# Routing tokens to experts: one-hot slots shared with ScalarE, row ids by thirds, low halves and put rows moved behind the row ids, and a weight load issued at a step's end

## What is computed

```
logits = (x2 / |x2|) @ (emb / |emb|).T / tau          # 3072 x 8
expert_idx = argmax(logits, axis=1)
gate_w = softmax(logits)[n, expert_idx[n]]
for e in range(8):
    mask = expert_idx == e
    h = maximum(x2[mask] @ w1[e], 0)                  # 384 -> 1024
    out[mask] = gate_w[mask, None] * (h @ w2[e])      # 1024 -> 384
```

## Time and profile before

| | us |
|---|---|
| median of 3 runs | 843.85 |
| lowest and highest run | 841.52, 848.44 |
| the profiled execution's own time | 842.68 |
| span of its profile | 840.9 |

### The profile page before, as it was taken

One profiled execution on the slowest core, in us unless ns is written; L12 is line 12 of the kernel. 1 busy time (PEld: TensorE's weight loads), 2 busy tenths in 40 slices (PEclk: granted clock), 3 DMA queues, 4 the chain that ended last, 5 costly groups with the idle time before them and its releaser, 6 DMA issues. The chain is left out here.

```text
span 840.9 us, 18148 instructions
## 1 busy us (share of the span) xinstructions
PE 819.6 (97%) x5840; PEld 745.6 (89%) x5841; DVE 641.4 (76%) x983; ACT 506.7 (60%) x1057; POOL 217.4 (26%) x239
## 2 busy tenths in 40 slices
PE   8999989999999999999999999898999999999995
PEld 7777768889999999999999998798999999999994
DVE  8999859999998998998998997824546464647552
ACT  5766777767667667666666766224545463646652
POOL 6434534321111111111111331123223222232111
PEclk9999999999999999999999999988999999999998
DMA  9999943225234234324323675299596769693440
GB/s 231 269 271 304 300 120 95 66 85 177 101 108 154 87 108 154 100 87 144 118 100 126 226 256 207 94 321 392 197 332 236 269 223 389 246 350 119 177 161 9
DMA packets 86141, 157.89 MB, mean 188 GB/s; under 512 B 8027, under 2 KB 23533, under 8 KB 86096
## 3 DMA queue, kind: packets, MB, share of 16 engines
q1 hardware_dynamic: 58384, 100.82, 36.9%
q10 hardware_dynamic: 23744, 45.69, 15.2%
q0 software_dynamic: 3968, 10.82, 3.5%
HBM read 117.97 MB, written 40.70 MB: 189 GB/s over the span
## 5 line engine op out<-in xcount | busy, mean ns | idle before, releaser
L1306 POOL TENSOR_TENSOR ew_l<-ew_raw,ew_h 128x512 fp32r<-128x512 f32 x48 | 62.4, 1300 | 272.3 <-DVE poly L1524 268.0
L1226 PE MATMUL y_ps<-wout_h,g_h 128*128 128x392 f32 x384 | 130.9, 341 | 0.4 <-DVE g_l L1515 0.4
L1227 PE MATMUL y_ps<-wout_l,g_h 128*128 128x392 f32 x384 | 130.4, 340 | 0.0
L1228 PE MATMUL y_ps<-wout_h,g_l 128*128 128x392 f32 x384 | 130.3, 339 | 0.0
L1226 PE MATMUL h_ps<-xT_h,win 128*128 (+1 forms) x288 | 113.4, 394 | 1.2 <-DVE diff L1505 0.9
L1701 DVE SCALAR_TENSOR_TENSOR ex_hT_l<-e_bank,ex_hT_h 128x512 fp32r<-128x512 f32 x48 | 33.2, 692 | 105.6 <-ACT ex_hT_h L1957 105.6
L1228 PE MATMUL h_ps<-xT_h,win 128*128 (+1 forms) x288 | 113.3, 394 | 0.0
L1227 PE MATMUL h_ps<-xT_l,win 128*128 (+1 forms) x288 | 112.8, 392 | 0.0
L1858 PE MATMUL e_bank<-ex_xT_h,w_ex 128*128 128x256 f32 x288 | 83.4, 290 | 3.1 <-issue 3.1
L1524 DVE COPY_PREDICATED poly<-large,diff 128x512 f32<-128x512 uint8 x96 | 72.0, 750 | 17.5 <-DVE poly L1520 17.5
L1859 PE MATMUL e_bank<-ex_xT_l,w_ex 128*128 128x256 f32 x288 | 83.0, 288 | 0.0
(11 more groups left out here) (244 smaller groups left out, 1992.8 us busy)
## 6 DMA issues: line engine op xcount, KB each, us to landing
w_raw<-in_w ACTq DMA_DIRECT2D x26, 1536.0 KB, 11.2
ew_raw<-in_w SPq DMA_DIRECT2D x48, 256.0 KB, 2.7
w_h<-ew_h SPq DMA_DIRECT2D x48, 256.0 KB, 2.3
w_l<-ew_l SPq DMA_DIRECT2D x48, 256.0 KB, 2.0
w_ex<-w_h SPq DMA_DIRECT2D x8, 1536.0 KB, 7.3
w_ex<-w_l SPq DMA_DIRECT2D x8, 1536.0 KB, 12.8
kv_sb<-in_kv SPq DMA_DIRECT2D x24, 384.0 KB, 6.4
krT_sb<-in_krT SPq DMA_DIRECT2D x44, 192.0 KB, 6.5
```

Of the source, the lines that this page charges most:

```text
L1226: pe.matmul(out, lh, rh, start=start, stop=False)
L1227: pe.matmul(out, lh, rl, start=False, stop=False)
L1228: return pe.matmul(out, ll, rh, start=False, stop=stop)
L1306: pool.tensor_tensor(ew_l[:, slot, :], raw, ew_h[:, slot, :].bitcast(F32), ALU.subtract).then_inc(ew_l_made, 1)
```

## The change

The diff, cut to what the text speaks of:

```diff
-        GROUP = 8
+        GROUP = NT // 3
+        apart = poly[:, :, :].rearrange("p a f -> p (a f)")[:, 0:GROUP * P].rearrange("p (n s) -> p n s", n=GROUP)
...
+            act.activation(table_in[:, :], bias[:, 0:1], ACT.Exp, scale=0.0)
+            act.wait_ge(slot_made, 1)
+            for n in range(2 * GROUP, NT):
+                far = act.activation(apart[:, n - 2 * GROUP, :], row128[:, :], ACT.Square, bias=slot[:, n:n + 1], scale=-1.0)
+            far.then_inc(last_hot, 1)
+            act.wait_ge(last_hot, 1)
+            act.activation(oh_slot[:, 2 * GROUP:NT, :], apart[:, :, :], ACT.Relu, bias=ones[:, 0:1],
+                           scale=-2.0).then_inc(last_hot, 1)
             act.wait_ge(w1_loaded[0], 16)
             for n in range(SPLITS):
                 cols = slice(n * STEP, (n + 1) * STEP)
                 act.activation(unit_h[:, cols], unit_raw[:, cols], ACT.Copy).then_inc(w1_high, 1)
-            act.wait_ge(shifted, 1)
-            act.activation(ex[:, :, :], below[:, :, :], ACT.Exp).then_inc(ex_made, 1)
+                if n == 0:
+                    act.wait_ge(shifted, 1)
+                    act.activation(ex[:, :, :], below[:, :, :], ACT.Exp).then_inc(ex_made, 1)
...
-            keep_warm(pe, h_ps[1], ident, 24)
-            pe.wait_ge(ids_placed, 1)
-            for n in range(NT):
-                pe.wait_ge(slot_hot, n // GROUP + 1)
-                last = pe.matmul(id_ps, oh_slot[:, n, :], rhs_id[:, n, :], start=(n == 0), stop=(n == NT - 1))
+            keep_warm(pe, h_ps[1], ident, 21)
+            for third in (0, 2, 1):
+                pe.wait_ge(ids_placed, 1 if third == 0 else 2)
+                if third == 2:
+                    pe.wait_ge(last_hot, 2)
+                else:
+                    pe.wait_ge(slot_hot, third + 1)
+                for n in range(third * GROUP, (third + 1) * GROUP):
+                    last = pe.matmul(id_ps, oh_slot[:, n, :], rhs_id[:, n, :], start=(n == 0), stop=(n == 2 * GROUP - 1))
             last.then_inc(ids_turned, 1)
-            keep_warm(pe, h_ps[1], ident, 15)
+            keep_warm(pe, h_ps[1], ident, 8)
...
-                                     op0=ALU.mult, op1=ALU.add).then_inc(r_dve, 1)
-            done[0] += 1
-            step(dve.tensor_tensor(in_tile[:, :, :], wide(tile_of[:, 1, :], COLS),
-                                   group_at[:, :].unsqueeze(1).to_broadcast([P, NT, COLS]), ALU.is_equal))
-            dve.tensor_tensor(rhs_id[:, :, :], in_tile[:, :, :], wide(ids[:, :], COLS), ALU.mult).then_inc(ids_placed, 1)
-            for n in range(0, NT, GROUP):
-                dve.tensor_tensor(oh_slot[:, n:n + GROUP, :], wide(slot[:, n:n + GROUP], P),
+                                     op0=ALU.mult, op1=ALU.add).then_inc(slot_made, 1)
+            def ids_of(at, end):
+                step(dve.tensor_tensor(in_tile[:, at:end, :], wide(tile_of[:, 1, at:end], COLS),
+                                       group_at[:, :].unsqueeze(1).to_broadcast([P, end - at, COLS]), ALU.is_equal))
+                dve.tensor_tensor(rhs_id[:, at:end, :], in_tile[:, at:end, :], wide(ids[:, at:end], COLS),
+                                  ALU.mult).then_inc(ids_placed, 1)
+            def slots_of(at):
+                dve.tensor_tensor(oh_slot[:, at:at + GROUP, :], wide(slot[:, at:at + GROUP], P),
                                   row128[:, :].unsqueeze(1).to_broadcast([P, GROUP, P]),
                                   ALU.is_equal).then_inc(slot_hot, 1)
-            for n in range(SPLITS - 1):
-                unit_low(n)
+            ids_of(0, GROUP)
+            dve.wait_ge(slot_made, 1)
+            slots_of(0)
+            ids_of(GROUP, NT)
+            slots_of(GROUP)
...
-            unit_low(SPLITS - 1)
...
+            unit_low(0)
...
+        def find_rest(dve, settle):
+            settle(dve.tensor_scalar(empty[:, :], table[:, :], 0.0, float(ALL + 1), ALU.is_equal, ALU.mult))
...
+            settle(dve.tensor_reduce(solo_of[:, :], passed[:, :, :], AX.X, ALU.add))
...
-                sp.wait_ge(gates_turned, 1)
+                sp.wait_ge(gates_made, 1)
...
+                unit_low(0, 0, 1)
                 for t in range(2):
                     x_low(0, t)
+                unit_low(0, 0, 2)
+                find_rest(dve, settle)
                 take_gates()
...
+                def first_block(high, low):
+                    ps = h_ps[0][:, 0:PAIR]
+                    cols = [slice(a * FE, a * FE + P) for a in range(KD)]
+                    pe.wait_ge(w1_high, SPLITS)
+                    pe.wait_ge(xT_high, 2)
+                    for a in range(KD):
+                        pe.matmul(ps, high[:, cols[a]], xT_h[:, a, :], start=(a == 0), stop=False)
+                    for a in range(KD - 1):
+                        pe.wait_ge(w1_split, a + 1)
+                        pe.matmul(ps, low[:, cols[a]], xT_h[:, a, :], start=False, stop=False)
+                    pe.wait_ge(xT_split, 2)
+                    for a in range(KD):
+                        pe.matmul(ps, high[:, cols[a]], xT_l[:, a, :], start=False, stop=False)
+                    pe.wait_ge(w1_split, SPLITS)
+                    pe.matmul(ps, low[:, cols[KD - 1]], xT_h[:, KD - 1, :], start=False, stop=True)
...
                     hidden_high(u)
-                    load_pair(u + 2, par)
                     if is_first(u):
+                        act.wait_ge(gates_made, 1)
                         load_solo(0)
+                    else:
+                        load_pair(u + 2, par)
...
                         finish(u, 1)
+                        if is_first(u):
+                            load_pair(u + 2, par)
```

42 lines of the change are left out of this document (24 added, 18 removed).

## The result

| | before | changed |
|---|---|---|
| median of 4 runs each, same chip | 842.83 | 835.36 |
| lowest and highest | 841.52, 848.44 | 833.43, 836.9 |
| the profiled execution's own time | 842.68 | 833.43 |
| span of its profile | 840.9 | 831.7 |

The ratio is 0.9918 [0.9889, 0.9948], which is 6.9 us; the medians differ by 7.5. The two profiled executions differ by 9.2 us, where the sum said 9.5. The profiled execution of the changed kernel is the fastest of its runs, so this close agreement is partly luck; why the medians show less comes under e7 to e12.

A forecast was written before the change was run, and what follows sets the result against it. PE bounds the kernel, so its idling or half clock before 600 us counts. Route 3.5 plus third unit's load 6.0 gave 9.5 us off the profile's 842.7: 833.2, with 1.2 for the median 834.4; range 831.5 to 840.5.

The forecast's parts named there:

- The route up to the row ids: Slots split between DVE and ACT: `get_row` at 535.4 instead of 537.92, 2.5 us earlier.
- The gates: Behind `get_row`: gates' columns end at 538.85, a low half at 540.05, PE's gate matmuls at 539.6.
- The gathers: POOL's two gathers start at 536.5 and 537.95, the last lands at 541.85; if both are slow, 0.8 later.
- The end of the route's block: Block ends about 540.05, PE could begin the next at 540.9, rows turned at 542.35: 3.5 us saved.
- The first block's last low half: DVE, behind the barrier: ends at 544.7, covered by PE's work; without that cover it costs 1.2 at most.
- The solo's issues: ACT in step 0: the two load issues take 0.4 to 0.5 us each, high halves begin 4.0 us earlier.
- The first rival: The solo's second issue still holds ACT 4.1 us: only 0.3 us won there, 840.0; chance 1 in 10.
- Step 1: PE's 3.1 us idle at its start and 2.9 us of low clock go: 6.0 us saved.
- The third unit's weights: Issued at 565.3, landing about 582.3; PE feels only what lands after 584.1.
- The rival that ends slower: Third unit's weights too late for step 1: 849.8, 5 in 100; partial delay about 839, another 5.
- The median: Whole kernel: 834.4, from 833.2 plus 1.2 for the runs; faster by over 1% 0.52, within 0.44.
- The thin route: Row ids later, squares at 0.35, both gathers slow: route saves 1.9, 836.0, or 836.6 with longer low clock; 15 in 100.

The follow-up runs named there:

- e7: The changed kernel itself, run again without edits: 836.70 against 841.97 for the kernel before, ratio 0.9935.
- e12: e11 with 3 more filler matmuls between the first and second group of id matmuls: 834.63 against 841.94 for the kernel before, ratio 0.9916.
- e1: The kernel before with only the third unit's load moved to the end of step 0: 838.96 against 843.44, ratio 0.9947.
- e6: The changed kernel with all three thirds of the one-hot slots on DVE again: 837.41 against 841.97 for the kernel before, ratio 0.9938.
- e8: The changed kernel with the filler ahead of the gate matmuls back to 15 from 8: 834.87 against 842.65 for the kernel before, ratio 0.9899.
- e10: The changed kernel with filler of 3 in the id matmuls' wait and 4 behind the first gate matmuls: 834.63 against 842.65 for the kernel before.
- e11: e8 with the third unit's load issued between the first unit's x half and its last block: 834.99 against 841.94 for the kernel before.
- e2: The changed kernel with the third unit's load back ahead of the solo's: 839.74 against 843.44 for the kernel before, ratio 0.9952.
- e3: The changed kernel with the third unit's load issued right behind the solo's two: 839.40 in one execution.
- e4: The changed kernel with the second of two gathers issued at the next block's start: 842.04 against 843.44 for the kernel before, ratio 0.9981.
- e5: The changed kernel with filler for 8 matmuls behind the first gate matmuls: 836.18 against 841.97 for the kernel before, ratio 0.9920.
- e9: The changed kernel with three filler matmuls between the first two thirds of the id matmuls: 836.39 against 842.65 for the kernel before, ratio 0.9921.

## Why the prediction was right, point by point

- **The route up to the row ids: right.** `get_row` at 535.33 (forecast 535.4), the id matmuls' end at 535.06 (535.0). A square took 0.30 us, between the two bounds of 0.22 and 0.36, and not the 0.25 taken (eight began 0.30 apart; one lasts 0.39, as they overlap); the Relu took 1.15, not 1.0. The sixteen matmuls behind it took 0.12 each instead of 0.135, which made up for it.
- **The gates: right.** Their columns end at 538.75 (538.85), the low half at 539.88 (540.05), PE's gate matmuls at 539.83 (539.6).
- **The gathers: right by the row.** 536.46 and 537.91, as forecast, with 1.15 and 1.19 us: neither slow. The Trainium skill's rule ("SBUF — State Buffer", Who interferes with whom) would have made both slow as it was applied. Set beside DVE's rows, it fits better than the text gave it credit for. In the kernel before and in e1 the gather of 1.97 us begins 0.08 us behind a low half of 1.22 us; in the changed kernel and e6 the second gather begins during a column instruction of 0.55 and takes 1.18 to 1.19. The next block's first gather takes 1.42 us where a low half of 1.23 has 0.60 left (changed), and 0.94 where DVE does nothing (before). So it looks as if only what is left of the one DVE instruction under way counts. No run was made to test this.
- **The end of the route's block: the one step that failed, by 0.8 us.** The prediction let PE begin the next block 0.85 us behind the block's other engines (540.9), and counted the gather's landing (541.85) as a wait inside the next block, beside the barrier. The table shows that the next block begins only 0.5 to 0.6 us behind that landing. The landing came earlier than forecast (541.1), the barrier's share came on top, so PE began at 541.69; and the six turns ran at half clock, 1.34 us for 0.85. The rows were turned at 543.03, not 542.35, and unit 0 began at 545.25, not 544.5. This term was 0.7 too good. The low clock, which was taken "as before", ended at 549 instead of 552.6 and covered 3.75 us of unit 0's first product instead of 4.7: 0.5 back. So the route's sum of 3.5 came out as 3.3 in this execution. In e7's it came out as 1.6: the prediction priced a change of the low clock behind the barrier (a loss of 0.6, a gain of 2.3), but none ahead of it, where e7 has it from 534 on.
- **The first block's last low half: covered**, as counted, at half clock; at full clock (e8, e10, e11, e12) it costs 0.5 us, within the 1.2 that the prediction named.
- **The solo's issues: right.** 0.98 us together. The first rival (the second issue blocks all the same) is out: e1 and the changed kernel show two short ones, e2 and e3 that the third blocks.
- **Step 1: right.** No idle of PE at its start, clock 1.00. Of the 6.0 us, 5.9 came in the profile, and 5.2 in e1's.
- **The third unit's weights: right on the landing** (583.57, forecast 582.3), on its margin (PE would feel it from 584.1: at 583.57 it didn't) and, as far as e11 bears it out, on the reason, the same bytes at the same rate. The rival that ends slower did not come whole, but a small part of it did, and more often than the 5 in 100 that it was given: of eleven profiles with the late load step 1 is as short as before in four (changed, e4, e6, e7) and 0.7 to 2.5 us longer in seven (e1, e5, e8 to e12). The margin of 0.5 in the first profile was partly luck.
- **The median: 1.0 off, the saving by 2.** The profile's own time is 0.2 from the forecast, but it is that of the fastest run, and the addition of 1.2 for the runs was too small. The forecast took 9.45 us off a median of 843.85; measured are 7.5 off 842.83, and 5.3 in e7's batch. The kernel before came out 1.0 faster than it was taken for, which hid half of the miss. At 0.8% the saving is not the "faster by over 1%" that had 0.52, but the "within" that had 0.44. e7 shows a part of why: the changed kernel has the clock low for 11 us around the route in one profile (535 to 538.5 and 541.5 to 549) and for 17.5 in the other. Its ten executions spread over 5.5 us. That the clock makes all of this spread isn't shown, and e12 speaks against it: two of its executions have the same mean clock of 0.993 and take 834.34 and 837.91. A late start of the route and late weights in step 1 are the other two causes that the profiles show.
- **The thin route**, 836.0 to 836.6, is near e7's median of 836.7, but not by its mechanism: squares and gathers were fast there, the clock was low.

## What to carry to other kernels

Ask not only what an issue on an engine's queue moves but how closely it follows other large ones: with loads of 1536 KB the third within 7 us held ScalarE for 2.3 to 4.9 us. Moving whichever is needed last behind the engine's urgent work gained 5.9 us in every profile, since the same bytes landed at nearly the same time. Count what waits for it too: here the earlier start of everything else left the moved load up to 2.5 us late. Where a block ends in a gather, count the next block from the gather's landing plus the barrier, and let the other engines end by then; a gather pushed into the next block lands beside its big loads and costs more. Filler on TensorE at such a place can't be priced by its length: cutting it let the block end sooner and kept the clock low longer, and the times show no difference. Before explaining a difference between two medians of some 2 us, cut the profiled spans at fixed places, as in the table under e12: one execution can lose that much in a part that nobody edited.

## What the runs showed of the hardware

- A gather of 128 rows lands 3.2 to 3.4 us from its start with little DMA beside it (share 0.05 from 534 to 541 us in e8), 3.9 and 4.0 us where its instruction itself is 0.8 longer (before, e1), and 6.9 us beside a load of 1536 KB and the next block's other gathers (e4).
- The third load of 1536 KB on ScalarE's queue within 7 us of the first holds ScalarE for 4.10 us (before), 4.47 (e2), 4.88 (e3) and 2.31 (e11); 9.0 us behind the first it takes 0.39, with both earlier loads not yet landed (changed).
- The granted clock fell to half during or behind the id matmuls of 32 columns, though PE went on working: from 534 to 541 us it is busy 7.00 of 7.00 us in e7 and e8 and the clock of the stretch is 0.53. In e12, as busy and with three filler matmuls between the id thirds, it is at 1.00. Being busy alone did not keep the clock up here. e9 has the same three and its clock fell all the same, and e12 came to this place 2.3 us later, so the exact cause stays open.
- The Trainium skill ("TensorE: Matmul & The Clock Gate", What's actually happening) says that the point at which the clock changes varies from run to run. The traces agree: in two executions of one program the clock falls at 535 and at 534, and comes back at 538.5 in the one and only behind 551 in the other (e7).
- ScalarE does small activations back to back: eight over 128 columns take 2.45 us, one beginning each 0.30 us; five over 48 columns took 1.22, and one alone over 192 took 0.36.
